# Chunked recurrence with delta rule on one core: one product for v and u in `uv_r`, and scaled inputs loaded in three parts

## The reference

```python
for t in range(S):
    y[:, :, t] = np.einsum('bhd,bhde->bhe', rt, state)
    Sa = np.einsum('bhde,bhe->bhd', state, at)
    state_decay = state * wt[:, :, None, :] - np.einsum('bhd,bhe->bhde', Sa, bt)
    state = state_decay + np.einsum('bhd,bhe->bhde', vt, kt)
```

## Time and profile before

| | |
|---|---|
| median of 3 runs | 1001.37 us |
| profiled execution | 1005.59 us, span 1003.9 us |
| TensorE products | 826.9 us busy, 82% |
| weight loads | 603.9 us, 60% |
| VectorE | 556.5 us, 55% |
| ScalarE | 312.4 us, 31% |
| GpSimd | 252.2 us, 25% |
| mean granted clock | 0.935 |

### The profile page before, as it was taken

One profiled execution on the slowest core, in us unless ns is written; L12 is line 12 of the kernel. 1 busy time (PEld: TensorE's weight loads), 2 busy tenths in 40 slices (PEclk: granted clock), 3 DMA queues, 4 the chain that ended last, 5 costly groups with the idle time before them and its releaser, 6 DMA issues.

```text
span 1003.9 us, 27604 instructions
## 1 busy us (share of the span) xinstructions
PE 826.9 (82%) x11872; PEld 603.9 (60%) x11872; DVE 556.5 (55%) x1235; ACT 312.4 (31%) x739; POOL 252.2 (25%) x524
## 2 busy tenths in 40 slices
PE   2318988897998978859998789997899987899977
PEld 2218888897887978844454555455544545554555
DVE  8686667767776653125436635347355366353464
ACT  3102222223222222212225532235422255312354
POOL 1075856687776876000000000000000000000000
PEclk9999787898777888789999999999999999999999
DMA  3525455565656536232000000100000000000000
GB/s 102 137 57 115 96 131 127 131 147 112 137 121 132 133 73 159 60 101 81 10 31 7 21 14 1 40 1 21 14 7 30 10 12 17 14 1 0 1 21 20
DMA packets 125336, 61.31 MB, mean 61 GB/s; under 512 B 105120, under 2 KB 118048, under 8 KB 123296
## 3 DMA queue, kind: packets, MB, share of 16 engines
q1 hardware_dynamic: 95172, 32.61, 14.5%
q10 hardware_dynamic: 30044, 26.94, 10.4%
HBM read 45.37 MB, written 14.16 MB: 59 GB/s over the span
## 4 chain that ended last, share of the span: by engine, by line
PE 66%; DVE 15%; DMA 7%; ACT 6%; issue 4%; SPq 2%; ACTq 1%; DVEq 0%
PE ps_all L737 9%; PE ps_all L721 8%; PE ps_scan L103 4%; PE ps_all L778 4%; DMA l_by_unit<-l_blocks 3%; PE ps_all L854 3%; PE ps_all L815 3%; PE ps_scan L194 3%; ACT probs L914 3%; PE ps_scan L174 3%; PE ps_all L833 3%; PE ps_all L731 3%; PE ps_all L845 2%; PE ps_all L724 2%; DVE t_update_first L314 2%
## 5 line engine op out<-in xcount | busy, mean ns | idle before, releaser
L314 POOL TENSOR_TENSOR t_update<-l_by_unit,t_by_unit 128x133 f32<-128x133 f32 (+13 forms) x251 | 118.0, 470 | 131.8 <-DVE t_by_unit L316 64.4
L316 POOL TENSOR_TENSOR t_by_unit<-t_by_unit,t_update 128x133 f32<-128x133 f32 (+13 forms) x251 | 128.8, 513 | 19.7
L103 PE MATMUL ps_scan<-decayed_a_and_eye,scaled_then_x 40*128 40x104 f32 x768 | 67.8, 346 | 55.9 <-DVE decayed_a_and_eye L346 55.9
L721 PE MATMUL ps_all<-scaled_then_x,inputs_then_w_up 128*128 128x384 f32 x256 | 91.0, 499 | 15.7 <-DMA scaled_then_x<-y_t 10.0
L103 PEld LDWEIGHTS ps_scan<-decayed_a_and_eye,scaled_then_x 40*128 40x128 f32 x768 | 62.7, 252 | 57.9 <-DVE decayed_a_and_eye L346 42.3
L1005 DVE TENSOR_REDUCE minus_max<-ps_all 128x1 f32<-128x128 f32 (+5 forms) x96 | 54.9, 618 | 75.2 <-PE ps_all L819 75.2
L737 PE MATMUL ps_all<-gated,w_down 128*128 128x384 f32 x256 | 91.1, 499 | 0.0
L721 PEld LDWEIGHTS ps_all<-scaled_then_x,inputs_then_w_up 128*128 128x128 f32 x256 | 48.7, 194 | 52.2 <-issue 12.0
L880 ACT ACTIVATE h<-ps_all 128x384 f32<-128x384 f32 x64 | 28.0, 490 | 148.7 <-PE ps_all L724 148.7
L737 PEld LDWEIGHTS ps_all<-gated,w_down 128*128 128x128 f32 x256 | 46.0, 189 | 44.6 <-issue 19.1
L951 DVE TENSOR_SCALAR conv<-h,w_conv 128x768 f32<-128x768 f32 x32 | 19.9, 621 | 94.7 <-ACT h L880 94.7
(11 more groups left out here) (115 smaller groups left out, 1519.2 us busy)
## 6 DMA issues: line engine op xcount, KB each, us to landing
inputs_then_w_up<-in_x ACTq DMA_DIRECT2D x46, 321.4 KB
r_t_and_v_t<-in_rv ACTq DMA_DIRECT2D x48, 160.0 KB
l_by_unit<-l_blocks SPq DMA_DIRECT2D x24, 256.0 KB, 5.0
uv_and_ruv<-in_v ACTq DMA_DIRECT2D x48, 80.0 KB, 3.0
y_t<-y_out SPq DMA_DIRECT2D x24, 160.0 KB
out<-out_rows SPq DMA_DIRECT2D x24, 160.0 KB, 1.8
l_blocks<-ak_and_l SPq DMA_DIRECT2D x96, 32.0 KB, 2.0
t_blocks<-t_by_unit SPq DMA_DIRECT2D x24, 128.0 KB, 4.7
```

The source lines that it names most:

```text
L103: last = nc.tensor.matmul(PS[:, o:o + ROWS], weights, AL[c % NK][rows(h), p, :], start=True, stop=True)
L314: return (lambda: eng.tensor_tensor(tmp[:, 0:cols, 0:rest], l[:, s:s + 1, s + 1:BLK].broadcast_to(shape), t[:, 0:cols, s:s + 1].broadcast_ ...
L316: lambda: eng.tensor_tensor(t[:, 0:cols, s + 1:BLK], t[:, 0:cols, s + 1:BLK], tmp[:, 0:cols, 0:rest], ALU.subtract))
L721: nc.tensor.matmul(bank[n][:, 0:HALF], WIN[:, t, cols], XT[:, t, n * HALF:(n + 1) * HALF], start=(t == 0), stop=False)
```

## The change

`uv_r` no longer makes four products per place with weights of 64 columns. A new tile `VU` has, for each pair, three slots of 64 columns: v, u, v. Half 0 has its v in slot 0 and half 1 in slot 2, and u is written to slot 1 for both. So slots h and h+1 are (v, u) for half 0 and (u, v) for half 1, a contiguous weight of 128 columns whose product covers all 128 output partitions. `u_t` is gone; ScalarE writes u into `VU`. r and v are loaded by four DMAs a step in place of two, r into its own tile and v in pieces of 64 numbers into the slots.

The scaled inputs are loaded in three parts with a semaphore each: `w` of step c+1 after `x_rhs`, `a` of step c after `y_block`, k and b (`kb`) of step c+1 after `x_rhs2`, where c = n + GA. VectorE waits for each part where it reads it.

```diff
+PARTS = {"w": slice(0, WCOLS + 1), "a": slice(WCOLS + 1, WCOLS + 1 + HC), "kb": slice(WCOLS + 1 + HC, XCOLS)}
...
-    RV = [sb(f"r_t_and_v_t{n}", [ROWS, 2, P8, C]) for n in range(3)]
-    RT = [RV[n][:, 0, :, :] for n in range(3)]
-    VT = [RV[n][:, 1, :, :] for n in range(3)]
+    RT = [sb(f"r_t{n}", [ROWS, P8, C]) for n in range(3)]
+    VU = [sb(f"v_u_v_t{n}", [ROWS, P8, 3, C]) for n in range(3)]
...
-    UT = sb("u_t", [ROWS, P8, C])
...
             pe.wait_ge(m["ut_sb"], n + 1)
-            pe.wait_ge(m[f"r{n % 3}"], 32 * (n // 3 + 1))
+            pe.wait_ge(m[f"r{n % 3}"], 64 * (n // 3 + 1))
...
             for p in range(P8):
                 for h in range(2):
-                    nc.tensor.matmul(PH[h][own(h), seg(p, C)], VT[n % 3][rows(h), p, :], RT[n % 3][rows(h), p, :],
-                                     start=True, stop=True)
-                for h in range(2):
-                    last = nc.tensor.matmul(PH[h][own(1 - h), seg(p, C)], UT[rows(h), p, :], RT[n % 3][rows(h), p, :],
-                                            start=True, stop=True)
+                    vu = VU[n % 3][rows(h), p, h:h + 2, :].rearrange("r k t -> r (k t)")
+                    last = nc.tensor.matmul(PH[h][:, seg(p, C)], vu, RT[n % 3][rows(h), p, :], start=True, stop=True)
...
-        def load_x(c):
+        def load_x(c, part):
             if c >= 2:
                 act.wait_ge(m["prepped"], c - 1)
             for h in range(2):
-                act.dma_start(INX[c % 2][rows(h), :], in_x[c, h]).then_inc(m[f"inx{c % 2}"], 16)
+                act.dma_start(INX[c % 2][rows(h), PARTS[part]], in_x[c, h][:, PARTS[part]]).then_inc(m[f"{part}{c % 2}"], 16)
...
-                act.dma_start(RV[n % 3][rows(h), :, :, :].rearrange("r k p t -> r (k p t)"),
-                              in_rv[n, h].rearrange("r k p t -> r (k p t)")).then_inc(m[f"r{n % 3}"], 16)
+                act.dma_start(RT[n % 3][rows(h), :, :], in_rv[n, h, :, 0]).then_inc(m[f"r{n % 3}"], 16)
+                act.dma_start(VU[n % 3][rows(h), :, 2 * h, :], in_rv[n, h, :, 1]).then_inc(m[f"r{n % 3}"], 16)
...
-        load_x(1)
+        for part in ("w", "kb", "a"):
+            load_x(1, part)
...
+            soon, next_up = 2 <= n + GA < NT, 2 <= n + GA + 1 < NT
             if live: move(XS, PX, "x", "x_sb", n)
+            if next_up: load_x(n + GA + 1, "w")
             if live: move(YS, PY, "y", "y_sb", n, -1.0)
-            if 2 <= n + GA + 1 < NT: load_x(n + GA + 1)
+            if soon: load_x(n + GA, "a")
             if ahead: bkn_move(c)
             if live: move(ZS, PX, "e", "z_sb", n)
+            if next_up: load_x(n + GA + 1, "kb")
             if live: u_move(n)
...
-                nc.scalar.activation(UT[:, :, :], by8(PU, C)[0:ROWS], ACT.Copy, scale=-1.0).then_inc(m["ut_sb"], 1)
+                nc.scalar.activation(VU[n % 3][:, :, 1, :], by8(PU, C)[0:ROWS], ACT.Copy, scale=-1.0).then_inc(m["ut_sb"], 1)
...
-            dve.wait_ge(m[f"inx{c % 2}"], 32 * (c // 2 + 1))
+            dve.wait_ge(m[f"w{c % 2}"], 32 * (c // 2 + 1))
...
         def bk(c):
+            dve.wait_ge(m[f"kb{c % 2}"], 32 * (c // 2 + 1))
...
         def al(c):
+            dve.wait_ge(m[f"a{c % 2}"], 32 * (c // 2 + 1))
...
-        for h in range(2):
-            sp.dma_start(INX[0][rows(h), :], in_x[0, h]).then_inc(m["inx0"], 16)
+        for part in ("w", "kb", "a"):
+            for h in range(2):
+                sp.dma_start(INX[0][rows(h), PARTS[part]], in_x[0, h][:, PARTS[part]]).then_inc(m[f"{part}0"], 16)
```

More of the change, by code:

```diff
@@ L72, in recurrence @@
              "solved pool_chain set_eye consts set_inx set_dve set_pool arrived go "
-             "inx0 inx1 v0 v1 v2 r0 r1 r2 l_out0 l_out1 l_in t_out t_in0 t_in1 stored0 stored1")
+             "w0 w1 a0 a1 kb0 kb1 v0 v1 v2 r0 r1 r2 l_out0 l_out1 l_in t_out t_in0 t_in1 stored0 stored1")
     m = {n: sem("r_" + n) for n in names.split()}
```

## The result

The kernel after takes 1033.51 us (median of 4 runs, 1031.35 to 1040.79), the kernel before 1002.41 in its 4 runs beside it: a ratio of 1.0345, 95% interval 1.0299 to 1.0392. **It is 3.45% slower**; forecast were 1024 us and a range of 1002 to 1040. The profiled execution of the kernel after took 1034.76 us (span 1033.0, mean granted clock 0.902 where it was 0.935).

The account below looks back on a forecast made before the run. No engine alone bounds the recurrence: a chain of TensorE products, L-block transfer and issue does. Terms 18.4 + 3 + 1 + 0 + 1.5 - 1.6 = +22.3 us gave 1024 us, range 1002 to 1040.

Parts of the forecast that it names:

- Part A: `uv_r` product on TensorE: +0.97 us a step on 19 chain steps, +18.4 us, plus 3 for phases at the lower clock.
- The rival of the moving columns: `uv_r`: moving columns set the price, 1.21 us a phase; 1012 us in all, chance 0.17.
- that of the number of products: `uv_r`: product count sets the price, 0.91 us for 32 records; about 1008 us, chance 0.08.
- The three `uv_r` at the lower clock: Recurrence: three `uv_r` phases run at the lower granted clock, one more us each, +3 us.
- Part B: ScalarE's queue after `u_t`: four r and v issues mostly hidden, +1 us; up to 10 if Part A costs nothing.
- Part C: Scaled inputs loaded in three parts: six issues in place of two, placed where ScalarE is free; no cost.
- Part D: Transfers, the L-block load on the loop: smaller v pieces against, half of `in_x` gone for; 0, ends +8 and -27 us.
- the rival's 24 us: L-block load lands 3 us sooner on 8 turns, -24 us; chance 0.09 of 981 us, 0.08 of about 1000.
- Part E: Kernel start: `a` of chunk 3 queues behind other loads, moving the first elimination about 1.5 us; +1.5, between -1 and +4.
- Part F: TensorE issue stalls on the chain: 64 of 768 records fewer a step, -1.6 us, between 0 and -3.
- The third rival: Both steps of a turn become critical, all 24 `uv_r` count: +32 us, queue +5, 1040 us; chance 0.13.
- The turn: One turn of the recurrence's loop, two steps, 30.6 us before: about 31.6 us if the forecast is right.

Follow-up runs that it names:

- 4: Kernel after with 104 moving columns in place of 64 in `uv_r`, the surplus overwritten by the next product: ratio 1.0118 to the kernel before.
- 5: Kernel before with all `uv_r` products of v issued first, then all of u, so two quarters of the array run abreast: ratio 1.0048.
- experiment 1: Kernel before with only the scaled inputs loaded in three parts; `uv_r` and the r and v loads unchanged: ratio 1.0007.
- 3: Kernel after with all its loads, but `uv_r` again as four products of 64 weight columns a place: ratio 1.0102 to the kernel before.
- 11: Kernel after with 104 moving columns in `uv_r` and 64 in `first_blocks` and `all_blocks`: 1004.82 us against 1004.27, ratio 1.0017 to the kernel before.
- 9: Kernel before with `first_blocks` and `all_blocks` at 64 moving columns in place of 40: ratio 0.9989.
- 6: Kernel before with the gram product as 32 products of 64 weight columns, four quarters abreast, in place of 16 with 128: ratio 0.9986.

## Why the prediction was right, and where it was not

**The direction** was right for the reason given: the product's weight columns set its pace, and most of its phases are on the chain. **The size**, 22 us forecast and 31 measured, came as near as it did partly by luck: the clock had no term, the queue's was too small, and the largest, the phase's, was too big.

**Part A** took 1.97 us a phase; measured are 1.93 to 2.00. That the weight and not the moving columns decides, argued from L103 against L194, is shown by 4 and 5. Of the overlap on entering 0.07 us is left, from 0.2, as priced. What was too big is the count: `uv_r` was to be on the chain in 19 or more iterations, and it is in 16. The term, 18.4 + 3, stands against 14.0 us, the difference of the pieces on the two chains; two phases at the lower clock, not three, cost 1.7 us more each. The rival of the moving columns is out by 4. So is that of the number of products: by the Trainium skill, TensorEngine Tiling (Array Packing), Performance Considerations (Instruction Overhead), each product carries some 60 cycles of overhead. The prediction's estimate from this, 11 us gained by half the products, is not borne out by the trace, in which the phase went from about 1.15 to 1.93 us.

**The step that fell short is one that the sum took without a term: the same mean clock in the recurrence, 0.84, for both kernels.** The text named another clock as what no term foresees, and gave it nothing. It fell to 0.77, and an estimated 12 to 22 us go with it. The three `uv_r` at the lower clock count the slow time of the new phase alone, while the 52 us more at 1.2 GHz fell on all phases, and the gram product's share of the chain rose by 4.6 points.

**Part B** had +1 and is the term that was too small. In the kernel after the queue is hidden where TensorE runs at the full clock and v at its median: from the same timeline, `u_t`'s move at 177.99, four issues of 0.35 to 0.56 us, `x_rhs` at 181.90, ended by TensorE. Elsewhere it is not: TensorE waited 8.7 us for `x_rhs` in seven steps, up to 2.0 us each, where it had waited 0.5. That is 8 us for the +1, though not each of them need reach the end of the chain. With Part A undone, 3 has 16.7 us of such waits and 5 to 9 us of excess, so the bound of 10 us without cover was sound.

**Part C** is right: experiment 1 shows no cost. **Part D**'s 0 stands: the load landed 0.6 us sooner at the median, but TensorE was later than it, so nothing of the rival's 24 us could show. 11, with a faster TensorE, has the load on its chain again.

**Part E** is wrong in its mechanism. VectorE's timeline at the start:

```profile
40.87 0.69 DVE L348 TENSOR_TENSOR decayed_a_and_eye<-inputs_then_w_up,prefix_products 104x512 f32<-104x512 f32 x1 [6.15 <-DMA inputs_then_w_up<-in_x]
...
45.47 1.29 DVE L357 TENSOR_TENSOR ak_and_l<-ps_scan,mask_strict 128x512 f32<-128x512 f32 x2 [1.05 <-PE ps_scan L102]
46.68 0.18 DVE L314 TENSOR_TENSOR t_update_first<-l_by_unit,t_by_unit 128x31 f32<-128x31 f32 x1
```

The product did move behind the loads, but smaller parts land sooner, at 40.9 and not 42.4; the gram product is done by 45.5, a microsecond before the forecast's 46.4. The first elimination, at 46.68, comes 0.3 us later than before, and step 0 still begins 0.3 us earlier: nothing in place of +1.5.

**Part F**, -1.6, was in the right direction. TensorE's own waits for issue add up to 17.8 us before and 0.2 after; for the kernel before and then after, the longest in 70 to 440 us:

```profile
PE ps_scan L185 <- issue: 6.5, 7, 1.7
PE ps_scan L132 <- issue: 5.2, 5, 2.0
```

```profile
PE ps_scan L149 <- issue: 0.2, 1, 0.2
```

How much of the 17.8 had been on the chain, and so was saved, is open.

**The third rival**, both steps critical, 1040 us, is nearer in time and wrong in its reason: 16 iterations of `uv_r` are on the chain and not all 24. **The turn** was forecast at 31.6 us, 1.0 more than before; from step 7 to step 23 it is 32.0, which looks like a hit, but over the same steps it was 29.8 before, so it grew by 2.2.

Open: why the granted clock fell with the reshaped product, and in the last iteration; why the higher clock of 9 gained nothing; what in the loads costs, issues or pieces; and how the excess divides between the phase (14.0 us on the chain) and the queue (8.2 us more of waits), which together are as much as the excess or more. No run had the side-by-side product with neither the four issues nor a wide operand.

## What to carry to other kernels

Price a reshaped product by the row whose weight has the same columns, not by the count of products; then ask what the granted clock of its neighbours will be, since here that was a third to two thirds of the loss and showed on lines that nobody had edited. Where weights set a phase's pace, as in `uv_r`, a wider moving operand whose surplus is overwritten cost no time: try it when the clock row falls, and measure, since in the kernel before it gained nothing (9). Compare the list of waits before and after line by line: one wait that was 0.5 us and is 8.7 is a term of its own. And before a difference of one per cent is explained, set the runs against their clock, and say which runs the slope rests on.

## What the hardware showed unexpectedly

Widening products that need no widening made the kernel after faster: 104 for 64 moving columns, 1.0345 to 1.0118 at an unchanged 1.93 us a phase; 40 to 64 in two other phases, to 1.0166; both, to 1.0017, with the clock of the stage at 0.77, 0.84, 0.83 and 0.91. In the kernel before, widening the same two phases raised the clock and not the speed. An issue on ScalarE's queue took 0.42 us at best and 1.20 at worst for the same r load (L259), while ScalarE's compute waits behind it. And TensorE's waits for its own issue went from 17.8 us to 0.2 with 8% fewer records; with `uv_r` in quarters again they are 13 us (3), and the gram product in quarters has 9.2 us of them in front of it alone (6).
